# Splitting the first mixed output inside the expert attention, and one MLP weight split ahead of the drain

## The reference

```
x  = local + global attention over 8 heads of 64          # q, k, v given
x  = sum over 4 experts e of gate_e * (softmax(causal(x wq_e (x wk_e)^T)) x wv_e) wo_e   # best 2 of 4 experts per row
u  = x + (x^T U V)^T                                       # U 768x32, V 32x768: mixes rows of the sequence
out = u + relu(u w_ch1) w_ch2                              # width 2048 inside
```

## Time and profile before

| what | us |
|---|---|
| median of 3 runs | 458.41 |
| lowest, highest | 457.63, 460.41 |
| the profiled execution | 458.41 |
| its span in the profile | 456.6 |

### The profile page before, as it was taken

One profiled execution on the slowest core, in us unless ns is written; L12 is line 12 of the kernel. 1 busy time (PEld: TensorE's weight loads), 2 busy tenths in 40 slices (PEclk: granted clock), 3 DMA queues, 4 the chain that ended last, 5 costly groups with the idle time before them and its releaser, 6 DMA issues.

```text
span 456.6 us, 8488 instructions
## 1 busy us (share of the span) xinstructions
PE 442.3 (97%) x3194; PEld 368.0 (81%) x3194; DVE 190.8 (42%) x616; ACT 167.1 (37%) x452; POOL 173.1 (38%) x243
## 2 busy tenths in 40 slices
PE   4999999999999999998999999999999999999996
PEld 3677777887787887767998888888888888888885
DVE  5799989455632733544352222212223122222112
ACT  4888788232553654656430111110112111111102
POOL 2667766924961365775212122222112111222210
PEclk9999999999999999999999999999999999999999
DMA  8899950110020011110102011111111032311003
GB/s 257 257 244 298 299 161 1 51 45 2 1 94 0 2 47 47 47 48 1 47 10 61 24 46 46 41 31 46 47 46 47 0 93 92 93 46 47 25 1 138
DMA packets 29949, 33.47 MB, mean 73 GB/s; under 512 B 9204, under 2 KB 19444, under 8 KB 29908
## 3 DMA queue, kind: packets, MB, share of 16 engines
q1 hardware_dynamic: 29474, 32.40, 24.0%
q10 hardware_dynamic: 434, 0.52, 0.3%
HBM read 29.77 MB, written 3.15 MB: 72 GB/s over the span
## 4 chain that ended last, share of the span: by engine, by line
PE 89%; DVE 4%; issue 3%; ACT 2%; DMA 1%; SPq 0%; POOL 0%; DVEq 0%; ACTq 0%
PE ps_s L1220 27%; PE ps_o L1220 25%; PE ps_t L1220 12%; PE ps_s L1451 5%; PE ps_o L1484 4%; PE ps_t L1467 4%; PE ps_o L1272 3%; PE ps_s L1239 3%; PE ps_t L1252 3%; DVE probT L865 1%; PE ps_o L1396 1%; ACT prob L604 1%; DMA kT<-in_k 1%; DVE prob L847 1%; DVE smin L847 0%
## 5 line engine op out<-in xcount | busy, mean ns | idle before, releaser
L492 POOL TENSOR_TENSOR fl<-fraw,fh 128x512 fp32r<-128x512 f32 x32 | 41.4, 1292 | 177.9 <-DVE fh L1162 177.9
L604 ACT ACTIVATE prob<-prob,smin 128x256 f32<-128x256 f32 (+3 forms) x144 | 77.7, 540 | 36.4 <-DVE smin L847 36.0
L796 ACT ACTIVATE hidh<-ps_o 128x768 fp32r<-128x768 f32 x32 | 26.0, 813 | 175.9 <-PE ps_o L1220 175.9
L1203 DVE SCALAR_TENSOR_TENSOR hidl<-ps_o,hidh 128x768 fp32r<-128x768 f32 x32 | 30.7, 958 | 92.6 <-ACT hidh L796 92.6
L541 POOL TENSOR_SCALAR prob<-prob,sinv,one 128x256 f32<-128x256 f32 (+1 forms) x96 | 50.6, 542 | 22.4 <-DVE sinv L878 22.4
L567 POOL TENSOR_SCALAR prob<-prob,sinv,gate 128x128 f32<-128x128 f32 (+5 forms) x48 | 34.0, 717 | 51.6 <-DVE sinv L898 51.5
L1220 PE MATMUL ps_s<-hidh,fl 128*128 128x512 f32 x128 | 50.4, 394 | 0.0
L1220 PE MATMUL ps_s<-hidl,fh 128*128 128x512 f32 x128 | 50.2, 392 | 0.0
L1220 PE MATMUL ps_s<-hidh,fh 128*128 128x512 f32 x128 | 49.7, 388 | 0.0
L1162 DVE CAST fh<-fraw 128x512 fp32r<-128x512 f32 x32 | 14.4, 450 | 66.8 <-PE ps_t L1220 66.8
L1220 PE MATMUL ps_o<-xh,w_late 128*128 128x512 f32 (+1 forms) x160 | 41.6, 334 | 0.0
(11 more groups left out here) (182 smaller groups left out, 978.3 us busy)
## 6 DMA issues: line engine op xcount, KB each, us to landing
fraw<-in_w SPq DMA_DIRECT2D x32, 256.0 KB, 2.7
wraw<-in_w SPq DMA_DIRECT2D x8, 512.0 KB, 3.4
kT<-in_k SPq DMA_DIRECT2D x16, 224.0 KB, 4.1
vN<-in_v SPq DMA_DIRECT2D x8, 384.0 KB, 4.9
out<-prob SPq DMA_DIRECT2D x12, 256.0 KB, 2.8
qT<-in_q SPq DMA_DIRECT2D x7, 384.0 KB, 3.8
vB<-in_v SPq DMA_DIRECT2D x8, 192.0 KB, 4.8
kT<-in_k SPq DMA_DIRECT2D x7, 128.0 KB, 3.9
```

What stands on the lines that cost most here:

```text
L492: return pool.tensor_tensor(lo, raw, hi.bitcast(F32), ALU.subtract)
L604: act.activation(prob_s, prob_s, ACT.Exp, bias=smin[:, col:col + 1], scale=-1.0, accum_out=ssum[:, col:col + 1]).then_inc(done, 1)
L796: act.activation(hidh[:, f % 2, :], ps_o[:, 0:S], ACT.Relu).then_inc(hidh_done, 1)
L1203: dve.scalar_tensor_tensor(hidl[:, f % 2, :], ps_o[:, 0:S], 0.0, hidh[:, f % 2, :].bitcast(F32), ALU.max, ALU.subtract).then_inc(hidl_done, 1)
```

## The change

Two things are moved, nothing is added or removed. First, the three high copies of ACT go into its treatment of the "m" entries, straight after DVE's sum; the three low parts of DVE go one entry later each (piece 0 after sum 1, piece 1 after sum 2, piece 2 just ahead of `w01_lo(2)`), and all six leave the hand-over. Second, in the MLP loop of DVE `f_hi(f+2)` stands ahead of `drain_dve(0)` instead of behind it, which matters at f = 16 alone.

```diff
 # ACT, fill_hi(v, place)
+                    elif kind == "m":
+                        act.wait_ge(sum_done, x + 1)
+                        part, _ = mixed_part(x)
+                        act.activation(part(oph[0]), part(o32[:, 0, :, :]), ACT.Copy).then_inc(oph_done, 1)
 # ACT, hand-over
-            for n in range(OP_PIECES[0]):
-                first_mixed_hi(n)
             w01_hi(4)
 # DVE, fill_take(v, place)
                     if kind == "w":
+                        if x == W1_IN_FILL - 1:
+                            mixed_lo(OP_PIECES[0] - 1)
                         w01_lo(x)
...
                         dve.tensor_tensor(o, src, o, ALU.add).then_inc(sum_done, 1)
+                        if x:
+                            mixed_lo(x - 1)
 # DVE, hand-over
-            for n in range(OP_PIECES[0]):
-                mixed_lo(n)
             w01_lo(4)
 # DVE, MLP loop
+                if f and f + FR - 1 < B * FT:
+                    f_hi(f + FR - 1)
                 if f == FT:
                     drain_dve(0)
-                if f and f + FR - 1 < B * FT:
-                    f_hi(f + FR - 1)
```

More of the change, by code:

```diff
@@ L752, in _ @@
                     fill_hi(v, 0)
[L755 to L759, removed]
             def mixed_hi(pr):
```

## The result

The changed kernel took 463.05 us (median of 7 runs, 461.73 to 464.15), the kernel before 458.86 (7 runs): a ratio of 1.0081, 95% interval 1.0058 to 1.0103. Measured again later, on another occasion, it was 1.0054, interval 1.0032 to 1.0076. By the two intervals together it is slower by 1.5 to 4.7 us. That is within the 1% or so in which the prediction put it, but the median of 463.05 is above the range of 458.7 to 462.0; the later median, 461.69 beside 459.53 for the kernel before, is not. The profiled execution took 462.32, its span is 460.5, 3.9 us over the span before.

What follows compares the result with a forecast made beforehand. PE, busy 97% of the span, was taken to bound the kernel. Hand-over 0, expert attention 0.55 and turn of the batch 1.44 summed to 1.99 us on 458.41, giving 460.4 us, range 458.7 to 462.0.

Steps and rivals of the forecast that it cites:

- What bounds the kernel: Whole kernel: PE, busy 97% of the span, so the change acts only by ending or making a wait of PE.
- what leaves the hand-over: Hand-over before the MLP: ACT's three copies and DVE's three subtractions leave, PE has no idle time there; gain 0.
- What enters the expert attention: Iterations 19 to 22: of six moved instructions only piece 2's high part on ACT delays PE; cost 0.55 us.
- The meeting of DVE and POOL: Piece 0's low part on DVE meets POOL's scaling: 0 in the sum, 0.43 us in the range.
- second reckoning: Same meeting, by the skill's exclusion rule: the low part starts at 207.14 when POOL ends, `safe` 0.04 us late.
- the rival: Contention: piece 0's low part lengthens by 0.73 us beside POOL, PE 0.43 us later, time 460.83; chance 0.11.
- a sign of being wrong: A low part of DVE over 0.9 us long, which would move iteration 21.
- The turn of the batch: MLP, f = 16: DVE's drains fall behind f_hi(18), so PE's whole(1) starts 1.44 us later; bounds 1.29 to 1.54.
- The hand-over from DVE to PE: At the turn: 0.15 us from the end of DVE's first drain to the start of PE's whole(1).
- The sum: Whole kernel: 0 - 0 + 0.55 + 1.44 = 1.99 us slower, 460.4 us in all; chance 0.65.
- The rivals: Whole time: relief 456.5 (0.04), only the turn 459.85 (0.12), contention 460.83 (0.11), turn does nothing 458.96 (0.03), clock 468.8 (0.03).
- the falling clock: MLP behind the turn: the new idle time drops the granted clock to 1.2 GHz, 8.4 us more, 468.8; chance 0.03.

Runs made afterwards that it cites:

- one_drain_first: The kernel before, with f_hi(18) put between the first and second of DVE's drains at the turn of the batch; ratio 1.0023 (0.9997 to 1.005).

## Why the prediction was wrong

- **What bounds the kernel, and what leaves the hand-over: right.** PE was busy throughout the hand-over before and after; the relief of ACT and DVE brought nothing (1.16 us of lag ahead of it, 1.16 behind).
- **What enters the expert attention: right.** One instruction of six costs; the forecast was 0.55 us, the traces show 0.53, and taking that instruction away gives the 0.80 us wait back.
- **The meeting of DVE and POOL: it happens, and costs nothing.** The low parts of pieces 0 and 1 took 0.92 and 0.99 us beside POOL's scaling; in the hand-over before, with POOL idle, each took 0.69. The first ended at 208.32, 0.54 after the end of POOL's scaling (206.26 + 1.52 = 207.78), the second at 212.01, 0.53 after it (211.48). Both thus look held until POOL ended. The prediction's second reckoning, in which the low part starts when POOL has ended, gives 207.78 + 0.69 = 208.47 for the first, 0.15 more than measured: it is close, not exact. The 0.73 us of the rival were too many. The cover, 0.55 us before, shrank to 0.20 and held: a low part of over 0.9 us, which the prediction named as a sign of being wrong that would move iteration 21, did come, and moved nothing.
- **The turn of the batch: right in mechanism and nearly in size.** 1.44 forecast, 1.35 measured. The hand-over from DVE to PE was priced too high: from the cast's start to PE's start took 350.66 - 349.58 = 1.08, where the sum had 1.17. The first drain began at 349.92, and such a drain alone lasts 0.68 (the row of `one_drain_first`), which leaves 0.06 for the hand-over, where the sum had 0.15.
- **The sum: this step failed.** It took PE's list behind a late start to last as long as before, and so put nothing there, without a reason. The traces show 1.36 us there: 0.11 in the first matmul behind the wait, and 1.25 in a slower pace of PE's matmuls with the clock at full, 0.08 a step. The change costs 0.53 + 1.35 + 1.36 = 3.24 us in the trace, where the sum had 1.99.
- **The base and the scatter: this took the median out of the range.** 458.41 + 3.24 = 461.7 would still lie inside it. But 458.41 was a low base: the kernel before came out at 458.86 over seven runs, and at 459.53 on the second occasion. The remaining 0.9 us of the first median (4.19 above its own base, not 3.24) stays unexplained; the second median was 2.16 above its base, as much too low. So the miss of the range was in part bad luck, and a hit with the second median, 461.69, would have been luck too, with the same step wrong.
- **The rivals.** None of them had this. The nearest, the falling clock, named the right place (what a wait does to the matmuls behind it) and the wrong cause: in the changed kernel the clock at the turn and behind it stayed at 1.00.

What stays open is what sets the pace. All three levels, 6.16, 6.24 and 6.31, have the granted clock at full; the difference lies in the start-to-start distance of the matmuls, which in the slow stretch of the kernel after is 0.120 us for 256 columns, and 0.113 in the same stretch before. The runs show that a wait of PE in the MLP brings the slower pace on; none tells what PE carries over from it, why it sometimes doesn't come, nor what ended it across a turn without a wait.

## What to carry to other kernels

Where one engine is the bound and busy, an instruction moved on another engine costs what stands behind it: look for the instruction behind it that the busy engine already waits for (here the one copy with no idle time ahead of it), and for an instruction that itself waits, since all behind it wait too (here a cast that can't start before PE ends, put ahead of a drain that PE needs). Price a new wait of PE above its own length: eight waits that the list gave as 4.7 us made the trace 10.0 us longer. To judge a change smaller than the scatter of the times, compare the distance between two instructions that lie around it: it repeated to 0.01 us here, while the medians of the unchanged kernel lay 1.7 us apart on one occasion (458.01 and 459.75). And a wait that is already in the profile is the place to look for a gain: there, not in the emptier lists elsewhere, lay the one step that helped.

## What the runs showed of the hardware that was not expected

- PE had three paces for the same matmuls at a granted clock of 1.00: MLP steps of 6.16, 6.24 and 6.31 us. Behind 16 breaks of 0.6 or 1.9 us the step was never 6.16; behind a wait at the turn it was 6.16 in two profiled executions of five and 6.24 in three; without a new wait it was 6.16 in all of seven.
- A wait in the list is shorter than the shift it makes. At the turn, 0.58 us listed made the next start 0.75 late and all behind it 0.86; 1.19 made 1.35 and, at the same pace, 1.46.
- Behind breaks of 1.93 us the granted clock fell to 1.2 GHz for 3.4 and 3.5 us in two cases of eight, and never behind those of 0.6 us; PE had been busy without a break for over 10 us ahead of each.
- DVE's subtraction of two SBUF tiles lasts 0.92 to 0.99 us beside POOL's scaling and 0.69 with POOL idle. Where DVE's started first (212.21, 0.67 us), the first of POOL's two scalings took 1.35 us, where it was 0.98 before. So each holds the other up, as the Trainium skill (SBUF — State Buffer, section Who interferes with whom) has it for two SBUF inputs.
